# Retention and two mixtures of experts on one core: attention inputs laid out by dimension and by position, K=64 score products, states summed in PSUM, x operands made from PSUM

## What is computed

```python
# attention: q, k, v are [2, 8, 768, 64]
gamma = 1.0 - 2.0 ** (-5.0 - np.arange(H)); scale = 1.0 / np.sqrt(D)
for t in range(S):
    state = gamma * state + einsum('bhd,bhe->bhde', k[:, :, t], v[:, :, t])
    y[:, :, t] = scale * einsum('bhd,bhde->bhe', q[:, :, t], state)
x = y.transpose(0, 2, 1, 3).reshape(1536, 512)
# first mixture, 8 experts, w1 [8, 512, 1024], w2 [8, 1024, 512]
P = exp(x @ w_gate - max); 8 times: P /= P.sum(1) + 1e-9; P /= P.sum(0) + 1e-9; P *= N / E
x = sum_e P[:, e:e+1] * (maximum(x @ w1[e], 0) @ w2[e])
# second mixture, 4 experts, gates p = probs / (probs.sum(-1) + 1e-9)
out = sum_e p[:, e:e+1] * (maximum(x @ w1[e], 0) @ w2[e])
```

## Time and profile before

| | us |
|---|---|
| three runs, median | 1603.11 |
| lowest, highest | 1601.84, 1603.68 |
| the profiled execution: its own time | 1601.33 |
| its span | 1599.5 |
| mean granted TensorE clock | 0.995 of full speed |
| PE, PEld, DVE, ACT, POOL busy | 1575.4, 1431.7, 895.3, 450.0, 96.5 |
| attention on TensorE ends, `up(0, 0)` begins | 76.7 |
| `logits` begins, `down(0, 0)` begins | 100.5, 109.3 |

### The profile page before, as it was taken

One profiled execution on the slowest core, in us unless ns is written; L12 is line 12 of the kernel. 1 busy time (PEld: TensorE's weight loads), 2 busy tenths in 40 slices (PEclk: granted clock), 3 DMA queues, 4 the chain that ended last, 5 costly groups with the idle time before them and its releaser, 6 DMA issues.

```text
span 1599.5 us, 21346 instructions
## 1 busy us (share of the span) xinstructions
PE 1575.4 (98%) x8248; PEld 1431.7 (90%) x8248; DVE 895.3 (56%) x1477; ACT 450.0 (28%) x848; POOL 96.5 (6%) x98
## 2 busy tenths in 40 slices
PE   9979999999999999999999999999999999999999
PEld 8878998998998899899889989988899889989988
DVE  6835785464555455554554654656546555555553
ACT  3422232232232133132222322334323213313221
POOL 4810000000000000000000000024100000000000
PEclk9999999999999999999999999999999999999999
DMA  9410010110110110100100101101011011010001
GB/s 198 89 53 27 27 53 4 50 53 1 53 53 0 52 43 9 52 26 26 52 26 26 52 0 53 53 1 53 0 53 53 1 53 53 0 52 28 25 32 74
DMA packets 67163, 64.64 MB, mean 40 GB/s; under 512 B 40608, under 2 KB 40736, under 8 KB 67104
## 3 DMA queue, kind: packets, MB, share of 16 engines
q1 hardware_dynamic: 54336, 61.08, 12.1%
q10 hardware_dynamic: 12768, 2.73, 0.9%
HBM read 60.67 MB, written 3.15 MB: 40 GB/s over the span
## 4 chain that ended last, share of the span: by engine, by line
PE 96%; DVE 2%; DMA 1%; POOL 1%; ACT 0%; issue 0%; SPq 0%; DVEq 0%; ACTq 0%
PE bank L1026 16%; PE bank L1027 16%; PE bank L1025 16%; PE bank L1004 14%; PE bank L1008 14%; PE bank L1006 14%; PE bank L894 1%; PE bank L922 1%; DVE w_lo L592 1%; PE bank L913 0%; PE bank L907 0%; DMA q_in<-in_q 0%; DMA w_raw<-in_moe_w 0%; PE bank L883 0%; POOL x_lo L319 0%
## 5 line engine op out<-in xcount | busy, mean ns | idle before, releaser
L1004 PE MATMUL bank<-x_hi,w_hi 128*128 128x384 f32 x1344 | 451.0, 336 | 7.5 <-POOL x_lo L319 3.7
L1008 PE MATMUL bank<-x_hi,w_lo 128*128 128x384 f32 x1344 | 450.6, 335 | 0.0
L1006 PE MATMUL bank<-x_lo,w_hi 128*128 128x384 f32 x1344 | 450.4, 335 | 0.0
L1027 PE MATMUL bank<-w_hi,h_lo 128*128 128x512 f32 x1152 | 449.1, 390 | 0.0
L1026 PE MATMUL bank<-w_lo,h_hi 128*128 128x512 f32 x1152 | 449.0, 390 | 0.0
L1025 PE MATMUL bank<-w_hi,h_hi 128*128 128x512 f32 x1152 | 448.5, 389 | 0.0
L761 DVE SCALAR_TENSOR_TENSOR acc<-bank,gate,acc 128x512 f32<-128x512 f32 x252 | 189.1, 751 | 374.9 <-PE bank L1027 374.9
L474 ACT COPY ups<-bank 128x384 f32<-128x384 f32 x288 | 138.8, 482 | 906.4 <-PE bank L1008 906.4
L706 DVE TENSOR_TENSOR ups<-bank,ups 128x384 f32<-128x384 f32 x288 | 155.4, 554 | 204.8 <-ACT ups L474 183.1
L1004 PEld LDWEIGHTS bank<-x_hi,w_hi 128*128 128x128 f32 x1344 | 253.0, 188 | 10.5 <-POOL x_lo L319 4.2
L1027 PEld LDWEIGHTS bank<-w_hi,h_lo 128*128 128x128 f32 x1152 | 216.2, 188 | 45.0
(11 more groups left out here) (84 smaller groups left out, 614.2 us busy)
## 6 DMA issues: line engine op xcount, KB each, us to landing
w_raw<-in_moe_w SPq DMA_DIRECT2D x48, 1024.0 KB, 5.0
k_in<-in_k SPq DMA_DIRECT2D x12, 256.0 KB, 3.6
q_in<-in_q SPq DMA_DIRECT2D x12, 256.0 KB, 4.5
v_in<-in_v ACTq DMA_DIRECT2D x10, 256.0 KB, 3.6
out<-acc SPq DMA_DIRECT2D x2, 768.0 KB, 4.4
out<-acc SPq DMA_DIRECT2D x6, 256.0 KB, 2.0
mask<-in_c_mask SPq DMA_DIRECT2D x1, 512.0 KB, 6.4
v_in<-in_v SPq DMA_DIRECT2D x2, 256.0 KB, 6.1
```

What stands on the lines that cost most here:

```text
L1004: nc.tensor.matmul(o, w1_hi[:, w, kc, fs], x_hi[:, x, kc, at], start=start and kc == 0, stop=False, skip_group_check=True)
L1006: nc.tensor.matmul(o, w1_hi[:, w, kc, fs], x_lo[:, x, kc, at], start=False, stop=False, skip_group_check=True)
L1008: last = nc.tensor.matmul(o, w1_lo[:, w, kc, fs], x_hi[:, x, kc, at], start=False, stop=kc == 1, skip_group_check=True)
L1027: last = nc.tensor.matmul(o, h_lo[:, f, b, rows], w2_hi[:, f, :], start=False, stop=(n == UC - 1))
```

## The change

The host hands over four arrays in place of three: q and k "by dimension" (`q_t`, `k_t`: for a chunk, row 64 r + d holds dimension d of the heads 2c + r, 128 positions each) and k and v "by position". Every load of a chunk is 128 rows of 2 KB. The host only rearranges; k is loaded twice.

- TensorE has no transposes in the attention. A score product takes 64 rows of `kt_in` and `qt_in`, alternately the rows 0 to 63 and 64 to 127, and writes to one of two banks by which half it reads.
- The decay is held in the tables: k is decayed to the middle of the sequence (`kdecay`, per chunk), q is raised by `rise` (`raise_q` on GpSimd into `q_up`), whose next chunk's table ScalarE makes (`rise_out`, 4 instructions of 128x128 for each of four chunks). The state is therefore a plain sum: the k v products are 8 matmuls of 64x64 outputs that add in the bank `ps_kv` over all chunks, and ScalarE copies the blocks into `state` (`state_out`, two 64x256 copies). The 8 VectorE instructions of `update_state` are gone, and so is `gout`.
- `mask` holds decay and scale, so y is final in PSUM. Three banks take y in turn. `x_high0`, `x_high1` (ScalarE), `x_sums`, `x_low0`, `x_low1` (VectorE) read it there; `x_sum` in SBUF holds the four sums; `sums_high` (ScalarE, 128x1024) and `sums_low` (VectorE for the chunks 0 to 3, GpSimd for 4 and 5, 128x1024) split them. GpSimd forms no sums any more.
- The second x stage uses the same functions: no copies to SBUF; sums on VectorE; `sums_low` on GpSimd. The third transposition in a `down` comes after its third group instead of its fourth.
- Inputs have two buffers per batch entry, scores and score banks two. TensorE's order is score(s + 1), attend(s). All attention loads are issued by SP; those of step s wait for the values product of step s - 4.
- `split_w1` and `w1_sums` of the first unit lie one step earlier or later in the VectorE and ScalarE lists (below), and `sums_high` of the last chunk leads the first unit's list on ScalarE, where before the high parts of the last chunk came after that unit's hidden values.

```diff
@@ score and attend on TensorE
-                for h in range(HEADS):
-                    last = nc.tensor.matmul(ps_scores[h // 4][:, h % 4 * P:(h % 4 + 1) * P], k_t[:, h // 2, h % 2, :],
-                                            q_t[b][:, h // 2, :], start=True, stop=True)
+                    for r in range(2):
+                        d = slice(HD * r, HD * r + HD)
+                        last = nc.tensor.matmul(ps_scores[s % 2][r][:, pair * P:(pair + 1) * P], kt_in[c % 2][b][d, pair, :],
+                                                qt_in[c % 2][b][d, pair, :], start=True, stop=True)
...
+                    for h in range(HEADS):
+                        d = slice(HD * (h % 2), HD * (h % 2) + HD)
+                        at = HD * (DC * b + h // 2)
+
+                        last = nc.tensor.matmul(ps_kv[d, at:at + HD], k_dec[b][:, h, :], v_in[c % 2][b][:, h, :],
+                                                start=False, stop=True, skip_group_check=True)
+                    last.then_inc(kv_done, 1)
...
-            transposes(0, 0, 0)
+            score(0)
             for s in range(STEPS):
-                c, b = s // BATCH, s % BATCH
-                score(s, b)
                 if s < STEPS - 1:
-                    transposes(s + 1, 1 - b, (s + 1) // BATCH)
-                attend(s, b, c)
+                    score(s + 1)
+                attend(s)
@@ the x operands on VectorE
+            def x_sums(n):
+                def sub(o, a, b):
+                    return nc.vector.tensor_tensor(o, a, b, ALU.subtract)
+
+                t1, t2, t3, t4 = [x_sum[:, 2 * i:2 * i + 2, :] for i in range(4)]
+                y0, y1 = x_bank(n, 0), x_bank(n, 1)
+
+
+                dve.wait_ge(x_b12, n + 1)
+
+                dve.wait_ge(x_hi1, n + 1)
+                then_wait(sub(t1, t3, y0[:, 0:2, :]))
+                then_wait(sub(t2, y1[:, 2:4, :], t1))
+                sub(t4, y0[:, 2:4, :], t2)
+                sub(t3, y1[:, 2:4, :], t3).then_inc(x_summed, 1)
+
+            def x_low0(n):
+                dve.wait_ge(x_hi0, n + 1)
...
@@ on GpSimd
+            for s in range(BATCH, STEPS):
+                raise_q(s)
+                if s < STEPS - BATCH:
+                    decay_k(s)
+            for n in range(CH - 2, CH):
+                sums_low(n)
@@ on ScalarE
+            for s in range(STEPS):
+                c, b = s // BATCH, s % BATCH
+                if b == 1:
+                    x_high0(c)
+                elif c > 0:
+                    x_high1(c - 1)
+                if c < CH - 1:
+                    state_out(s, b)
+                if b == 0 and c > 0:
+                    sums_high(c - 1)
+                if b == 0 and 2 <= c + 2 < CH:
+                    rise_out(c + 2)
+                if s == STEPS - 2:
+                    split_w1_high(0, 0, first=True)
+                if s == STEPS - 1:
+                    split_w1_high(0, 1)
```

More of the change, by code:

```diff
@@ L79, in retention_moe_moe_kernel @@
         w2_raw = w_raw[:, :].rearrange("p (c n) -> p c n", c=UC)
+        with ExitStack() as early:
+            mask = sb("mask", [P, 2, DC, P], F32, early)
+            rise = [sb(f"rise{r}", [P, DC, P], F32, early) for r in range(2)]
         w2_hi = sb("w2_hi", [P, UC, DM], F32R)
         w2_lo = sb("w2_lo", [P, UC, DM], F32R)
-        x2_tmp = sb("x2_tmp", [P, 14, P])
-        x2_y = [x2_tmp[:, 4 * b:4 * b + 4, :] for b in range(BATCH)]
-        x2_t = x2_tmp[:, 8:14, :]
-        logit_t = x2_tmp[:, 0:NSUB, :].rearrange("p i t -> p (i t)")
+        x_sum = sb("x_sum", [P, 4 * 2, P])
         ident = sb("ident", [P, P])
@@ new lines, in state_out, with rise_out @@
+            def state_out(s, b):
+                act.wait_ge(kv_done, s + 1)
+                for r in range(2):
+                    d = slice(HD * r, HD * r + HD)
+                    last = nc.scalar.copy(state[b][d, :, d],
+                                          ps_kv[d, b * DC * HD:(b + 1) * DC * HD].rearrange("p (c e) -> p c e", c=DC))
+                last.then_inc(state_ready, 1)
+            def rise_out(c):
+                if c == 2:
+                    act.wait_ge(rise_in, 32)
+                else:
+                    act.wait_ge(rise_ready, c - 2)
+                    act.wait_ge(q_raised, BATCH * (c - 2))
+                for pair in range(DC):
+                    last = nc.scalar.mul(rise[c % 2][:, pair, :], rise[(c - 1) % 2][:, pair, :], step[:, pair:pair + 1])
+                last.then_inc(rise_ready, 1)
@@ L477, in hidden_high, with unit @@
                 nc.scalar.activation(h_hi[:, f, b, :], src, ACT.Relu).then_inc(h_hi_ready, 1)
-            def unit(k, p, x2=None):
+            def unit(k, p, x2=None, sums=None):
+                if sums is not None:
+                    sums_high(sums)
                 for half in range(2):
@@ L493, in unit @@
                 if x2 is not None:
-                    x2_sums_high(x2)
+                    sums_high(x2)
                 for half in range(2):
```

534 lines of the change are left out of this document (249 added, 285 removed).

## The result

| | kernel before | changed kernel |
|---|---|---|
| median of the runs beside each other | 1603.39 us (4 runs) | 1574.03 us (4 runs, 1573.68 to 1578.24) |
| ratio | 1 | 0.9825, 95% interval 0.9807 to 0.9843 |
| profiled execution: own time / span | 1601.3 / 1599.5 us | 1574.2 / 1572.4 us |
| first matmul of `down(0, 0)` starts | 109.10 us | 84.79 us |
| from there to the end of the span | 1490.4 us | 1487.6 us |

The forecast was 1571 us, 1561 to 1586; the time is 1574.0. By the time alone this is as near to rival B (1577) as to the forecast; only the durations in the trace tell the two apart. The two lowest rows of the table split the 27.1 us by which the span shrank. Up to `down(0, 0)` the kernel gained 24.3 us, the forecast to the tenth. Behind it the gain is 2.8 us where 7.8 stood. (`down(0, 0)` is read here at its first matmul in the timeline.

A forecast was written before the change was run, and what follows sets the result against it. TensorE was taken as the bound, with gains only where it waits: 1601.3 less 24.3 us up to down(0, 0) and 7.8 at the second x stage gives 1569.2, and a median 1.8 higher, 1571 us; 8 in 10 from 1561 to 1586.

The forecast's parts named there:

- rival B: Attention scores: their loads do not overlap, scores stay at 1.98 us, step 5.0 us, time 1577 us; chance 0.27.
- The bound: Whole kernel: TensorE busy 1575 of 1599.5 us, so attention changes gain only where TensorE waits and before down(0, 0).
- The TensorE step: Attention step on TensorE: 5.66 us falls to 4.0, from 3.6 to 5.0, without transposes and with half-height scores.
- the sum: Whole kernel: profiled 1601.3 less 24.3 before down(0, 0) and 7.8 at the second x stage, 1569.2; median 1571 us.
- All three hide under 4.0: Middle attention steps: DVE 3.4 us, ACT 2.4 and POOL's two products of 1.07 fit under TensorE's 4.0 us step.
- Transfers: Attention loads: 1.05 MB per step instead of 0.79, binding only at the start, taken there at 250 GB/s.
- T: Time at which attention step 8 ends on TensorE: taken as 44.5 us, between computed 41.6 and 46.4.
- The chain behind T: Attention end to down(0, 0): DVE and ACT set the pace; up starts at 60.6, down(0, 0) at 85.0, 24.3 us less.
- The second x stage: Second x stage: two TensorE waits shrink to one of 0.9 us, clock recovers; 7.8 us less, from 4 to 9.
- C: Attention loads: transfers set the pace of every step, 1583 us at 200 GB/s, 1596 at 153; chance 0.10.
- D: Attention: all goes well, keys times values near 0.5 us, transfers near 400 GB/s, T near 38, 1564 us; chance 0.10.
- E: Attention: TensorE's clock falls to its lower level throughout, steps take 8.5 us, 1608 us, slower than before; chance 0.03.

The follow-up runs named there:

- e7: The changed kernel with keys-by-values products ordered heads 0, 2, 4, 6, then 1, 3, 5, 7, so the halves no longer alternate; 1574.26 us.
- e3: The changed kernel with ScalarE's multiplications for the next rise moved to the end of the following step, behind state_out; 1572.79 us.
- e4: The changed kernel with the first unit's four w1 sums on GpSimd instead of DVE, and w1 high and low parts reordered; 1571.50 us.
- e8: The changed kernel with e1, e3 and e4 together, plus reordered ScalarE and DVE work in the first unit; 1559.39 us.
- e1: The changed kernel with an unused tile grown by 2880 bytes, putting h_hi, h_lo, ups and acc at the addresses of the kernel before; 1568.75 us.
- e2: The changed kernel with each step's score products taking one half of the partitions after the other instead of in turn; 1578.82 us.
- e5: The changed kernel with 2880 unused bytes between h_lo and ups, so only ups and acc return to their earlier addresses; 1575.31 us.
- e11: The kernel of e8 with h_hi at 168448, a multiple of 512, instead of 170624; 1576.12 us.
- e12: The kernel of e8 with 128 unused bytes ahead of mask, rise, w2_hi and w2_lo, moving everything behind them too; 1559.11 us.

## Why the prediction was right, and where it was not

The time lay in the range and 3 us over the point. By its steps:

1. **The bound.** Right: TensorE is busy for 1553.9 of 1572.4 us, and the gain came from the stretch up to `down(0, 0)` and from the second x stage.
2. **The TensorE step, 4.0 us.** Right as a mean, by two errors that cancel. Scores 1.09 (1.0 forecast), state 1.09 with its change of form (0.9 + part of 0.2), values 0.98 (1.0). Keys times values measured 0.51 and not 0.9: the argument that the loads are those of the values product overlooked that their stream has 64 columns and that they too alternate; e7 puts 0.28 of the missing 0.4 on the alternation. So TensorE alone needs 3.67. Against it stood what the sum had at zero: from step 5 on, a wait of 0.6 us on DVE's x sums in every second step. Rival B had named waits around the y banks, with a late `x_high1`; the late piece was `x_high0`, behind `rise_out`, as e3 shows. "All three hide under 4.0" was right only on average: in one of two steps the chain of DVE and ScalarE is the later one. DVE's 128x1024 low part took 1.75 us and not 1.35, and POOL's products 1.3 each instead of 1.07 (lines L592, L312 and L325 below, means over 0 to 110 us). They are longer where they run at the same time: the low part at 47.70 us, with POOL idle for most of it, took 1.22.
3. **Transfers.** Taken at 250 GB/s, measured 318 from 0 to 20 us. TensorE waited 3.6 us for them, all in the first steps. T came at 43.7 instead of 44.5.
4. **The chain behind T.** Its places were right one by one, its sizes not. x sums ready at T + 11.9 (10.3): DVE began its low part 1.0 later, behind the last 0.6 us wait and ScalarE's high part, and the first of the w1 sums took 1.76 instead of 0.7, beside `raise_q` on POOL. The end of the attention at T + 15.9 (12.2): the same 1.6, and 2.1 of low clock, which was left out although the rule it needed (the clock falls behind a long wait) stood in the prediction itself. `up` at T + 17.2 (16.1), so 60.9 instead of 60.6. The second product's wait was then 0.6 instead of 2.6, since TensorE arrived later and slower. It was ready for this product 1.9 us late (64.6 us instead of 62.7), and a wait that had been forecast absorbed this. The copy itself came 0.7 us later behind T than forecast, and T 0.8 us earlier. That is why `down(0, 0)` was right to the tenth, and it was luck: the same order of work gave 84.8 to 88.5 in five executions, and in e4 and e8 each wait that goes calls up the next.
5. **The second x stage.** Right: one wait of 1.0 us on `acc` (0.9), the other gone, no low clock. Worth 7.8 by the forecast and 8.4 by the profiled executions of e1 and the kernel before.
6. **What was missing.** The sum had no term for work that the change does not touch. Moving `h_hi` by 2880 bytes cost 5.6 us over 288 `down` groups. In the profiled execution, 1569.2 us was forecast and 1574.2 measured: 5.6 of this, less the 0.6 that the second x stage gave above its forecast. The median then lay 0.2 below that execution and not 1.8 above it, so 3 us of the 5 are left between 1571 and 1574; these 2 us are chance. Nothing in the rows of before could show it; a look at the addresses beside the unused tile `place` could have raised the question.

Of the rivals, B (scores at 1.98) is out, and e2 shows that even without alternation the step would be 4.2 and not 5.0. C is out: 318 GB/s in the first 20 us, 331 in the next 10. D's conditions (keys times values near 0.5, faster transfers) were met in part, but T stopped at 43.7, not at 38. DVE's waits account for 1.2 us of that; the rest lies in the 3.6 us that TensorE still waited for transfers in the first steps, and in a step of 3.67 us. E is out: in the profiled execution the clock was low only behind the 4.3 us wait. Its argument that the clock falls only behind waits of 2.4 us and more does not hold in general: in e2 and e5 products ran slowly behind waits of 1.3 and 2.1 us in the first steps, and in e11 behind one of 2.1.

Means of the other engines' instructions in the changed kernel, 0 to 110 us (busy us, mean ns), against the earlier trace rows:

```profile
L312 POOL TENSOR_TENSOR k_dec<-k_in,kdecay 128x512 f32<-128x512 f32 x10 | 13.4, 1339 | 11.1 <-DMA k_in<-in_k 11.1
L325 POOL TENSOR_TENSOR q_up<-qt_in,rise 128x512 f32<-128x512 f32 x10 | 13.2, 1323 | 11.7 <-PE bank L931 11.2 <-DMA qt_in<-in_q_t 0.5
...
L592 DVE TENSOR_TENSOR x_lo<-x_sum,x_hi 128x1024 fp32r<-128x1024 f32 x4 | 7.0, 1746 | 0.0
```

## What to carry to other kernels

When a change alters the size of any tile in SBUF, read the addresses of the operands behind it and time the untouched inner loop in both profiles; here 64 bytes were worth 17 us, more than most edits. Halves of the array that take turns are worth their order, 0.55 us of 1.64 here; that each product loads while the other half runs is the likely reason, which no run shows by itself. And where TensorE stands at the end of a stage, follow the whole queue of the engine it waits for: in the profiled executions taking away the first wait gained 1.4 us, reordering what stood behind it, with the rise moved, another 7.7.

## What the runs showed of the hardware

- The time of one of `down`'s matmuls (128 rows, 512 columns) went from 0.227 to 0.234 us (2.72 to 2.81 us a group) with the distance of the loaded tile from the streamed one modulo 256 bytes: best at 0, worst at 96 of the five that were tried. `up`'s matmuls, whose operands did not move, stayed at 334 to 336 ns.
- Eight 64-row, 128-column products took 1.09 us with halves in turn, 1.64 with one half after the other, against 1.98 for full height.
- Eight 64-column products into alternating halves of PSUM took 0.51 us, 0.80 one half after the other.
- The length of a wait alone does not tell what the clock does behind it. Behind a wait of 4.3 us at step 11 products ran slowly in all five kernels that have it (granted clock 0.51 from 55 to 64 us in the changed one), and behind the 4.0 of e3 and the 3.6 of e7 and e4 too. Behind 1.5 us in e4 and 2.1 in e8 and e12 none did; behind the same 2.1 us in e11 two did (0.79 from 48 to 56 us).
- DVE's 128x512 sum took 1.76 us beside a GpSimd product and 0.69 alone, a 128x1024 low part 1.74 and 1.22; in e4 one took 3.4 us beside GpSimd's 2.7 us one. Even a 128x32 part (`wg_parts`) took 2.04 us, from 65.55 to 67.59 us, beside a GpSimd instruction that ended at 67.55; in the kernel before it took 0.18.
